# Causal masks of the routed attention: behind the expert outputs in steps 2 to 5, halves 1 to 7

## The reference, cut to what matters

```python
for e in range(E):                       # 4 experts, head width 64
    q, k, v = x @ wq[e], x @ wk[e], x @ wv[e]
    scores = scale * (q @ k.transpose(0, 2, 1))
    scores = np.where(causal, -1000000000.0, scores)
    scores = scores - scores.max(-1, keepdims=True)
    a = np.exp(scores)
    a /= a.sum(-1, keepdims=True) + 1e-09
    ye = a @ v @ wo[e]
    out += (weight of e for this token) * ye
```

## Time and profile before

| | us |
|---|---|
| median of 3 runs | 732.02 (731.32 to 732.1) |
| the profiled execution | 729.87 |
| its span, first to last instruction | 728.1 |
| PE busy in it | 693.2 (95%) |
| DVE busy in it | 388.2 (53%) |
| ACT busy in it | 321.7 (44%) |

### The profile page before, as it was taken

The page is one execution under the profiler, slowest core; times in us unless marked ns, Lnnn a source line. Parts: engine busy times, 40 slices in busy tenths (PEclk is TensorE's granted clock), DMA queues, the critical chain, the costliest instruction groups (busy, mean ns, idle before and its releaser), DMA issues.

```text
span 728.1 us, 12345 instructions
## 1 busy us (share of the span) xinstructions
PE 693.2 (95%) x4864; PEld 448.3 (62%) x4864; DVE 388.2 (53%) x773; ACT 321.7 (44%) x804; POOL 147.5 (20%) x179
## 2 busy tenths in 40 slices
PE   6996899999999999999999999999999999999998
PEld 6974555566656665566656665566665666555554
DVE  6997875365753846529364747445574323542200
ACT  2554446551465135662345424555146613554330
POOL 6763510034101601015110431003510000000000
PEclk9998999999999999999999999999999999999999
DMA  9996400002600070000710035000000000000000
GB/s 240 299 329 183 145 3 2 1 1 75 182 2 1 23 233 1 2 1 12 205 41 1 1 103 154 1 0 2 33 1 1 0 24 12 1 1 0 33 0 33
DMA packets 36921, 43.36 MB, mean 60 GB/s; under 512 B 2560, under 2 KB 27264, under 8 KB 36608
## 3 DMA queue, kind: packets, MB, share of 16 engines
q1 hardware_dynamic: 36864, 42.57, 19.8%
HBM read 37.84 MB, written 4.72 MB: 58 GB/s over the span
## 4 chain that ended last, share of the span: by engine, by line
PE 85%; DVE 6%; ACT 4%; issue 3%; DMA 1%; SPq 0%; DVEq 0%; ACTq 0%
PE bank L876 75%; PE bank L880 5%; PE bank L1037 3%; PE bank L1033 2%; ACT shared L431 2%; DVE idec L622 1%; DVE dec L613 1%; ACT k_sb L413 1%; DVE nmax L649 1%; DMA w_sb<-in_wT 1%; DVE att L682 1%; DVE shared L662 1%; DVE carry L620 1%; DVE idec L624 0%; DVE state L703 0%
## 5 line engine op out<-in xcount | busy, mean ns | idle before, releaser
L876 PE MATMUL bank<-wv_sb,k_sb 128*128 128x384 f32 x384 | 139.4, 497 | 0.0
L876 PE MATMUL bank<-xk_sb,wk_sb 128*128 128x384 f32 x384 | 138.1, 499 | 0.0
L649 DVE TENSOR_REDUCE nmax<-bank 128x1 f32<-128x128 f32 (+5 forms) x96 | 55.5, 620 | 92.2 <-PE bank L876 92.1
L876 PEld LDWEIGHTS bank<-xk_sb,wk_sb 128*128 128x128 f32 x384 | 68.4, 190 | 42.9 <-issue 5.5
L876 PEld LDWEIGHTS bank<-wv_sb,k_sb 128*128 128x128 f32 x384 | 67.5, 190 | 38.8 <-issue 3.7
L422 ACT ACTIVATE shared<-bank,nmax 128x128 f32<-128x128 f32 (+5 forms) x96 | 59.9, 629 | 52.4 <-DVE nmax L649 52.4
L357 POOL TENSOR_TENSOR state<-state,carry 112x512 f32<-112x512 f32 x20 | 24.8, 1238 | 263.4 <-DVE state L701 147.5
L880 PE MATMUL bank<-ident,shared 128*128 128x128 f32 x336 | 49.8, 280 | 20.9 <-ACT shared L431 10.3
L880 PEld LDWEIGHTS bank<-ident,shared 128*128 128x128 f32 x336 | 37.6, 141 | 43.7 <-ACT shared L431 14.6
L876 PE MATMUL bank<-xT_sb,wqk_sb 128*128 128x384 f32 (+1 forms) x240 | 63.9, 423 | 0.0
L452 ACT ACTIVATE att<-ident,bonus 128x128 f32<-128x128 f32 x192 | 58.7, 392 | 7.2 <-DVE bonus L629 7.2
(11 more groups left out here) (91 smaller groups left out, 989.5 us busy)
## 6 DMA issues: line engine op xcount, KB each, us to landing
rk_sb<-in_rk SPq DMA_DIRECT2D x24, 384.0 KB, 7.1
v_sb<-in_v SPq DMA_DIRECT2D x24, 256.0 KB, 7.5
w_sb<-in_wT SPq DMA_DIRECT2D x24, 227.5 KB, 5.5
r_sb<-in_rT SPq DMA_DIRECT2D x24, 224.0 KB, 5.1
k_sb<-in_kT SPq DMA_DIRECT2D x24, 224.0 KB, 6.5
out<-out_sb SPq DMA_DIRECT2D x24, 192.0 KB, 1.9
wk_sb<-in_w_k SPq DMA_DIRECT2D x1, 1536.0 KB, 12.0
wv_sb<-in_w_v SPq DMA_DIRECT2D x1, 1536.0 KB, 16.6
```

What stands on the lines that cost most here:

```text
L649: d.tensor_reduce(nmax[:, n:n + 1], scores(h, i, e)[:, 0:w], axis=AX.X, op=ALU.max, negate=True).then_inc(max_ready, 1)
L876: return nc.tensor.matmul(out, lhsT, rhs, start=start, stop=stop)
```

## The change

In halves 1 to 7 the two mask matmuls of steps 2 to 5 move from the end of the score matmuls to behind the expert outputs of step `i - 2`, ahead of the fill matmuls. In steps 0 and 1 they stay directly behind the scores, and so they do in all steps of half 0. No instruction is added or taken away, and the semaphore counts stay. `w - P` is the same column as `q0`.

```diff
@@ score_step(h, i)
                         mm(scores(h, i, e)[:, lo:hi], qk_sb[rows, m, q0:w], qk_sb[rows, QM + m, lo:hi], stop=hi != w)
+                if h == 0:
+                    causal(h, i)
+
+            def causal(h, i):
+
+                w = width(h, i)
                 for e in range(2):
-                    mm(scores(h, i, e)[:, q0:w], ident_b[:, :], later_b[:, :], start=False).then_inc(score_psum, 1)
+                    mm(scores(h, i, e)[:, w - P:w], ident_b[:, :], later_b[:, :], start=False).then_inc(score_psum, 1)
@@ attention_step(h, i, fill)
                 if i < STEPS:
                     score_step(h, i)
+                    if i < 2:
+                        causal(h, i)
                 for q in fill_a(i)[0] if fill else ():
                     mix(h - 1, q)
                 if 2 <= i < STEPS + 2:
                     output(h, i - 2)
+                    if i < STEPS:
+                        causal(h, i)
```

## The result

| | before | after |
|---|---|---|
| median | 731.70 us (731.32 to 732.10, 4 runs) | 749.89 us (746.79 to 752.62, 4 runs) |
| ratio | | 1.0251, 95% interval 1.0225 to 1.0278 |
| the profiled execution | 729.87 | 752.62 |
| its span, granted clock | 728.1, 0.993 | 750.9, 0.984 |

The change costs 2.5%, slower. The forecast was 749.6 us in 744.5 to 755.5.

A forecast was written before the change was run, and what follows sets the result against it. TensorE's queue was taken as the bound, with VectorE's chain equally long in odd halves; losses of 15.0 us (odd) and 2.6 (even), 17.6 together, on the 732.02 us median gave 749.6 us, range 744.5 to 755.5.

The forecast's parts named there:

- TensorE's queue is the time, VectorE's chain is equally long, both start at the mask: Attention steps of odd halves: TensorE's queue and VectorE's maxima and scaling, both from the mask, match within 0.14 us.
- The odd half, step by step: Steps 2 to 5: late masks delay transposes by 4.43 us, 0.67 returns; 3.76 us lost per odd half, 15.0 in four.
- back in third groups: Odd halves, steps 3 to 5: third transposes idle less for ScalarE's copy, giving back 0.30 + 0.25 + 0.12 us.
- The even half: Steps 2 to 5: shorter maxima leave slack, so only 0.86 us is lost per even half, 2.6 in three.
- The sum: Halves 1 to 7: odd halves' 15.0 plus even halves' 2.6 make 17.6 us lost.
- Unknown (1), outputs directly behind scores: Outputs on TensorE taken to start where the mask did; bounds +3.5 us at worst, -1.6 at best.
- The saved switch: Rival: one tiling-mode change less per step on TensorE, 28 x 0.10 = 2.8 us faster, 729.2 us; chance 0.03.
- The clock: Rival: new TensorE stalls in odd halves lower its granted clock, +16 us, 765.6 us; chance 0.03.

The follow-up runs named there:

- e5: Kernel before with odd halves' masks of steps 2 to 5 moved amid the outputs, behind the first two key tiles; 739.07 us, ratio 1.0109.
- e3: Kernel before with VectorE's scaling of the previous step put ahead of the step's maxima; 729.06 us, ratio 0.9948.
- e4: The changed kernel (after) with VectorE's scaling of the previous step put ahead of the step's maxima; 736.32 us, ratio 1.0050.
- e8: e7 with the masks of steps 2 to 5 behind the outputs as in the changed kernel; 732.40 us, ratio 1.0012 to before.
- e7: e3 with ScalarE's copies of the transposes ahead of the fill group's Relu and Square; 734.49 us, ratio 1.0042 to before.
- e10: e9 with late masks only in steps 2 and 3 of odd halves and 2 to 4 of even ones; 722.96 us, ratio 0.9868 to before.
- e1: The change kept in odd halves only, even halves as before; 749.68 us, ratio 1.0234 to before.
- e6: Kernel before with odd halves' masks of steps 2 to 5 behind the outputs and the fill matmuls too; 805.26 us, ratio 1.1017.
- e9: e7 with ScalarE's copies first only in steps 1 to 4, and between the two fill groups' Relus in odd halves' step 6; 725.90 us, ratio 0.9905 to before.

## Why the prediction was right

*TensorE's queue is the time, VectorE's chain is equally long, both start at the mask.* Right. The late mask became lateness of the transposes (holes ended by "DVE shared"), e5 scales it down, and e3 and e4 take it away by moving VectorE's scaling, with no change on TensorE.

*The odd half, step by step* (transposes' start after minus before, less what was lost earlier; half 1):

| | step 2 | step 3 | step 4 | step 5 | back in third groups | sum |
|---|---|---|---|---|---|---|
| forecast | 0.93 | 1.02 | 1.24 | 1.24 | 0.30 + 0.25 + 0.12 | 3.76 |
| measured | 0.94 | 1.07 | 1.24 | 1.24 | 0.25 + 0.19 + 0.07 | 3.98 |

The term that was most off is what comes back: 0.51 instead of 0.67, since the third groups stay idle for 0.24, not 0.19, and start 1.34 behind the first, not 1.28. The other 0.06 are in steps 2 and 3. Four halves: 15.9 instead of 15.0.

*The even half:* 0.67 measured, 0.86 forecast, three of them 2.0 instead of 2.6. The steps came as written (in half 2 the transposes of step 4 late by 0.34 more, of step 5 by 0.48 more, 0.19 of it given back between them); 0.1 less was lost in steps 2 and 3, since fill matmuls behind a mask let the transposes follow after 1.99 us and those behind outputs after 2.04, which the prediction had left out; and 0.1 came back in step 6's first fill group, whose next instruction followed after 2.03 us instead of 2.13. Why is open.

*The sum:* 17.6 forecast, 17.9 in the trace of halves 1 to 7: the odd halves were 0.9 too low and the even ones 0.6 too high. That the median, 749.89, lies within 0.3 us of the forecast is in part luck, as the four runs spread over 5.8 us.

*Unknown (1), outputs directly behind scores:* they start where the mask did (half 1: the scores' start to the outputs' 118.15 - 116.87 = 1.28, as to the mask before). No part of the bound was needed.

*The saved switch.* Real, but no rival in this kernel. The Trainium skill's rule (TensorEngine Tiling (Array Packing), Key Properties: a change of mode drains TensorE) agrees with e8 against e7, 0.14 us a step where neither waits. The earlier trace rows gave 0.10; the rest is the 0.05 by which the fill matmuls behind a mask are shorter (2.04 to 1.99). It pays once neither VectorE nor ScalarE is late, as in e10.

*The clock.* Not the cause of the loss: in halves 1 to 7 of after's profiled execution every window shows 1.00. But my argument against it was weak. I took from the earlier trace rows that holes as short as the new ones leave the clock up. In half 0 of after's own execution it was still full at 69 to 71 us, as in those rows, and fell right behind (below), and e1 shows one half with it. The chance of 0.03 was for a systematic fall, which only e6, with holes of 2.9 us and more, produced.

## What to carry to other kernels

When a producer is moved later in one engine's queue, look at what stands *behind its consumer* on the consumer's engine: here the larger part of an odd half's loss came from the scaling queued behind the late maxima, and 1.67 us were left when it no longer was. Two queues that run between the same two points and are equally long to within 0.14 us mean that any delay of the common start, beyond what work slips in between, is paid in full. And before an order is judged, the other engines' orders are worth a try: the move of all 28 steps costs 17.9 us with VectorE's maxima first, and brings 4 x 0.02 + 3 x 0.57 = 1.8 us from e7 to e8; kept to the 17 steps where nothing waits for it, it brings 0.3% from e9 to e10 (4 x 0.28 + 3 x 0.43 = 2.4 us in the traces).

## What the runs showed of the hardware

The traced executions differ by the granted clock, nearly all of it in half 0. The later halves of one kernel agree to 0.02 us in all traces but those of e1 (one half) and e6; half 0 ends (first gate matmul) anywhere from 97.40 us in e10 to 102.63 in after. Over 56 executions of the kernel before, beside the experiments, the time ran from 728.05 us at a mean clock of 0.998 to 735.35 at 0.986, the four at 0.984 at 734.2 to 735.1, the 14 at 0.988 at 731.7 to 733.7. After's four lie at 746.79 (0.995), 749.71 and 750.08 (0.988) and 752.62 (0.984): some 17 to 18 us above before at the same clock. Windows of 5 us in half 0 (engine busy us, then granted clock, DMA share, GB/s), before and then after, same instructions:

```profile
70.00:75.00 5.00, 2.91 (x22) 1.65 (x22) 3.69 (x12) 2.55 (x7) 0.00 (x0) 1.00 0.00 0
75.00:80.00 5.00, 3.85 (x83) 3.04 (x84) 4.96 (x5) 1.71 (x5) 0.51 (x1) 1.00 0.27 73
```

```profile
70.00:75.00 5.00, 3.90 (x22) 2.29 (x22) 3.31 (x11) 2.01 (x7) 0.00 (x0) 0.62 0.00 0
75.00:80.00 5.00, 4.32 (x68) 3.18 (x66) 4.96 (x5) 0.96 (x2) 0.00 (x0) 0.50 0.02 3
```

Before, TensorE is busy for 2.91 of 5 us at full clock; after, it is at 0.62 and then 0.50 (1.2 GHz), and the same 22 instructions fill 3.90. What preceded is nearly alike in both: full clock from 65 us on, and a hole of 1.47 us ahead of the transposes at 70.0 and 70.1; only further back do they differ (60 to 65 us: clock 0.64 before and 0.57 after). So in this stretch the clock held in one execution and fell in the other; a comparison by two single profiles can be 5 us off by it. That e3's profiled execution shows the fall too (a kernel faster than before) says that it doesn't come with the late masks. Whether a change elsewhere shifts how often it happens stays open.
